# Two fused kernels in one stream: tile loops kept in the program instead of unrolled, and the state update formed in its own buffer

## What is computed

```python
m_new = np.maximum(f_gate[:, :, t] + m, i_gate[:, :, t])
f_stab = np.exp(f_gate[:, :, t] + m - m_new)
i_stab = np.exp(i_gate[:, :, t] - m_new)
C = f_stab[:, :, None, None] * C + i_stab[:, :, None, None] * np.einsum('bhd,bhe->bhde', vt, kt)
n = f_stab[:, :, None] * n + i_stab[:, :, None] * kt
h_tilde = np.einsum('bhde,bhe->bhd', C, qt)
y[:, :, t] = o * h_tilde / denom        # denom = max(|n.q|, 1), o = sigmoid(o_gate)
```

```python
xn = x / rms * rms_g
x = (silu(xn @ w_gate) * (xn @ w_val)) @ w_out      # first MLP
h = x @ w_in
out = (np.maximum(h, 0) + alpha * np.minimum(h, 0)) @ w_out2   # second MLP
```

## Time and profile before

| | us |
|---|---|
| median of 3 executions | 503.93 |
| all three | 505.44, 503.92, 503.93 |
| the profiled execution, its own device time | 505.44 |
| its span | 503.6 |

### The profile page before, as it was taken

One profiled execution on the slowest core, in us unless ns is written; L12 is line 12 of the kernel. 1 busy time (PEld: TensorE's weight loads), 2 busy tenths in 40 slices (PEclk: granted clock), 3 DMA queues, 4 the chain that ended last, 5 costly groups with the idle time before them and its releaser, 6 DMA issues.

```text
span 503.6 us, 9124 instructions
## 1 busy us (share of the span) xinstructions
PE 482.7 (96%) x3161; PEld 463.4 (92%) x3161; DVE 317.4 (63%) x643; ACT 212.7 (42%) x508; POOL 233.9 (46%) x250
## 2 busy tenths in 40 slices
PE   5998989999999999999999999999999999998996
PEld 3887978998999999998999999999899999988996
DVE  7585897657787474449678556438779622236663
ACT  1441536245635324236545423234654422245552
POOL 3540748535657326143746334340855522225673
PEclk9998999999999999999999999999999999999999
DMA  6768332123434680003344390002342320004562
GB/s 112 163 135 176 105 103 75 44 59 98 119 85 116 113 119 2 2 0 74 121 96 91 115 167 1 1 2 56 93 117 81 90 66 0 1 5 114 135 126 97
DMA packets 80729, 41.23 MB, mean 82 GB/s; under 512 B 51548, under 2 KB 80684, under 8 KB 80684
## 3 DMA queue, kind: packets, MB, share of 16 engines
q1 hardware_dynamic: 80684, 40.65, 36.2%
HBM read 38.67 MB, written 1.97 MB: 81 GB/s over the span
## 4 chain that ended last, share of the span: by engine, by line
PE 78%; DVE 12%; issue 3%; POOL 3%; ACT 3%; ACTq 0%; POOLq 0%; DVEq 0%
PE bank L976 38%; PE bank L984 16%; PE bank L987 8%; PE bank L940 4%; PE bank L928 3%; PE bank L904 2%; PE bank L881 2%; PE bank L935 2%; POOL w L837 1%; DVE u L750 1%; PE bank L946 1%; DVE xn L711 1%; PE bank L918 1%; PE bank L919 1%; DVE win L720 1%
## 5 line engine op out<-in xcount | busy, mean ns | idle before, releaser
L845 POOL TENSOR_TENSOR hidT<-hid,hidT 128x384 fp32r<-128x384 f32 x112 | 118.3, 1057 | 227.7 <-ACT hidT L510 227.4
L510 ACT CAST hidT<-hid 128x384 fp32r<-128x384 f32 x112 | 57.5, 513 | 131.5 <-DVE hid L733 93.8
L976 PE MATMUL bank<-x2T,win 128*128 128x384 f32 x512 | 100.2, 339 | 1.2 <-ACT x2T L551 0.8
L976 PEld LDWEIGHTS bank<-x2T,win 128*128 128x128 f32 x512 | 87.6, 188 | 2.9 <-DVE win L720 1.3
L727 DVE SCALAR_TENSOR_TENSOR u<-th,bank 128x384 f32<-128x384 f32 x48 | 26.6, 554 | 92.0 <-ACT th L532 91.9
L976 PE MATMUL bank<-xT,wg 128*128 128x384 f32 x384 | 76.4, 342 | 1.8 <-DVE u L727 1.8
L976 PE MATMUL bank<-xT,wv 128*128 128x384 f32 x384 | 76.3, 341 | 0.0
L984 PE MATMUL bank<-w,hidT 128*128 128x320 f32 x384 | 68.2, 313 | 4.1 <-POOL w L837 3.5
L976 PEld LDWEIGHTS bank<-xT,wg 128*128 128x128 f32 x384 | 67.1, 191 | 2.9 <-issue 2.0
L976 PEld LDWEIGHTS bank<-xT,wv 128*128 128x128 f32 x384 | 66.7, 189 | 1.2 <-DVE hid L733 0.4
L984 PEld LDWEIGHTS bank<-w,hidT 128*128 128x128 f32 x384 | 59.2, 188 | 6.9 <-POOL w L837 5.7
(11 more groups left out here) (126 smaller groups left out, 631.4 us busy)
## 6 DMA issues: line engine op xcount, KB each, us to landing
shared<-in_moe_w_out SPq DMA_DIRECT2D x38, 320.0 KB, 4.9
shared<-in_moe_w_in SPq DMA_DIRECT2D x34, 256.0 KB
shared<-in_moe_w_in SPq DMA_DIRECT2D x34, 128.0 KB
q_in<-in_q SPq DMA_DIRECT2D x12, 160.0 KB, 4.4
k_in<-in_k SPq DMA_DIRECT2D x12, 160.0 KB, 4.8
v_in<-in_v SPq DMA_DIRECT2D x12, 160.0 KB, 4.8
o_in<-in_o_gate SPq DMA_DIRECT2D x12, 160.0 KB, 4.4
shared<-in_moe_w_gate SPq DMA_DIRECT2D x6, 256.0 KB
```

What stands on the lines that cost most here:

```text
L510: a.copy(hidT[:, i % NH, 0], hid[:, i % 2]).then_inc(s_hid_hi, 1)
L845: gp.tensor_tensor(hidT[:, i % NH, 1], hid[:, i % 2], hidT[:, i % NH, 0].bitcast(F32), ALU.subtract).then_inc(s_hid_lo, 1)
L976: last = te.matmul(dst, w[:, blk, col:col + P], x[:, part, xb, :], start=(n == 0), stop=(n == len(terms) - 1))
```

## The change

Two things are changed.

- The loop over t = 1, 2 of every engine, and SP's loops over m in `stream`, become loops of the program (`Fori`): the body is there once, a register holds t or m, and a branch at its end goes back to its start. Every semaphore value and DMA address in it that depends on t or m is computed in registers.
- A new step on DVE, at the place of `state`: `upd` is the bank A[2] times `pairmask`, a constant of ones on each pair's own half and zeros on the cross blocks. The bank is free after it (`s_upd`), and PE's `kT` and one `xT` wait for that instead of `s_C`. In `inter` one add of `upd` into C takes the place of the two adds that read the bank. Four memsets fill `pairmask`.

```diff
--- before.py
+++ after.py
@@ -171,6 +171,8 @@
         C = sb("C", [P, H, DA])
         tmp = sb("tmp", [P, H, DA])
         hsum = sb("hsum", [P, H, DA])
+        upd = sb("upd", [P, H, DA])
+        pairmask = sb("pairmask", [P, 2, DA])
         den = sb("den", [P, 3, H])
         xr = sb("xr", [P, H, D])
         xa = sb("xa", [P, H, D])
@@ -268,6 +270,7 @@
         s_intra_mm = sem("s_intra_mm")
         s_hsum = sem("s_hsum")
         s_state_mm = sem("s_state_mm")
+        s_upd = sem("s_upd")
         s_C_dec = sem("s_C_dec")
         s_C = sem("s_C")
         s_absn = sem("s_absn")
@@ -310,7 +313,7 @@
         s_load_win = [sem(f"s_load_win{p}") for p in range(2)]
         s_load_w2 = [sem(f"s_load_w2{p}") for p in range(2)]
         s_group = [sem(f"s_group{g}") for g in range(G)]
-        N_CONST, N_CONST_DVE, GATE_STEPS = 14, 12, 3 * G + 6
+        N_CONST, N_CONST_DVE, GATE_STEPS = 14, 16, 3 * G + 6
 
 
 
@@ -330,7 +333,7 @@
 
             walk(PROLOGUE, mlp, att, weights, None, 0)
             walk(FIRST, mlp, att, weights, 0, 1)
-            for t in range(1, NT - 1):
+            with eng.Fori(1, NT - 1) as t:
                 walk(MERGED, mlp, att, weights, t, t + 1)
             walk(EPILOGUE, mlp, att, weights, NT - 1, None)
 
@@ -409,7 +412,7 @@
 
             def stream(t):
 
-                for m in range(J2 // 4 - 1):
+                with sp.Fori(0, J2 // 4 - 1) as m:
                     for p in range(2):
                         load_w2(t, 2 * m + p, p)
                         load_win_behind(t, 2 * m + p, p, 2 * m + p + 2)
@@ -447,7 +450,7 @@
                 load_win(p, p)
             stream(0)
             store(0)
-            for t in range(1, NT - 1):
+            with sp.Fori(1, NT - 1) as t:
                 load_rows(t + 1)
                 for g in range(G):
                     load_group(t + 1, g)
@@ -601,6 +604,9 @@
             vec.memset(cap[:, ::HALVES], -BIG).then_inc(s_const_dve, 1)
             for r in (64, 96):
                 vec.memset(decay_lhs[r:r + H, :].bitcast(F32), 1.0).then_inc(s_const_dve, 1)
+            for r, one in ((0, 0), (REM, 1)):
+                vec.memset(pairmask[r:r + REM, one], 1.0).then_inc(s_const_dve, 1)
+                vec.memset(pairmask[r:r + REM, 1 - one], 0.0).then_inc(s_const_dve, 1)
             vec.memset(win[0:REM, :, NB, :].bitcast(F32), 0.0).then_inc(s_const_dve, 1)
             dve.wait_ge(s_const, N_CONST)
             vec.tensor_copy(identR[:, :], ident[:, :]).then_inc(s_const_dve, 1)
@@ -676,12 +682,9 @@
                     dve.wait_ge(s_gx, BACK + t + 1)
                     vec.tensor_tensor(tmp[:, :, :], heads(A[1]), wide(gx[:, 0, g], P, H, DA), ALU.mult).then_inc(s_tmp, 1)
                     vec.tensor_tensor(C[0:KP], C[0:KP], wide(gx[0:KP, 2, g], KP, H, DA), ALU.mult).then_inc(s_C_dec, 1)
-                    dve.wait_ge(s_state_mm, BACK + n + 1)
+                    dve.wait_ge(s_upd, n + 1)
                     dve.wait_ge(s_C_dec, n + 1)
-                    for half in range(2):
-                        own = slice(HP * half, HP * half + D)
-                        last = vec.tensor_tensor(C[own, half::2], C[own, half::2], heads(A[2])[own, half::2], ALU.add)
-                    last.then_inc(s_C, 1)
+                    vec.tensor_tensor(C[0:KP], C[0:KP], upd[0:KP], ALU.add).then_inc(s_C, 1)
                 elif what == "intra":
                     dve.wait_ge(s_intra_mm, BACK + n + 1)
                     dve.wait_ge(s_tmp, n + 1)
@@ -696,6 +699,11 @@
                     vec.tensor_scalar(den[:, 1, :], den[:, 0, :], 1.0, None, ALU.max).then_inc(s_den, 1)
                     dve.wait_ge(s_den, n + 1)
                     vec.reciprocal(den[:, 2, :], den[:, 1, :]).then_inc(s_rden, 1)
+                elif what == "state":
+                    dve.wait_ge(s_state_mm, BACK + n + 1)
+                    dve.wait_ge(s_C, BACK + n)
+                    vec.tensor_tensor(upd[0:KP, :, :].rearrange("p (a b) d -> p a (b d)", b=2), heads(A[2])[0:KP].rearrange("p (a b) d -> p a (b d)", b=2),
+                                      mid(pairmask[0:KP, :, :].rearrange("p b d -> p (b d)"), KP, PAIRS, 2 * DA), ALU.mult).then_inc(s_upd, 1)
                 elif what == "norm":
                     dve.wait_ge(s_rden, n + 1)
                     dve.wait_ge(s_xr, BACK + n + 1)
@@ -898,7 +906,7 @@
                     if what == "qT":
                         pe.wait_ge(s_x_lo, BACK + n - 2) if g == 0 else pe.wait_ge(s_tmp, n)
                     else:
-                        pe.wait_ge(s_gate_step, GATE_STEPS * (t + 1)) if g == 0 else pe.wait_ge(s_C, BACK + n)
+                        pe.wait_ge(s_gate_step, GATE_STEPS * (t + 1)) if g == 0 else pe.wait_ge(s_upd, n)
                     src, bank_ = (q_in, A[1]) if what == "qT" else (k_in, A[2])
                     for c in range(PAIRS):
                         last = te.transpose(bank_[0:KP, c * CH:(c + 1) * CH],
@@ -954,7 +962,7 @@
                     elif g == 0:
                         pe.wait_ge(s_tmp, G * t + G)
                     elif g == 1:
-                        pe.wait_ge(s_C, BACK + G * t + G)
+                        pe.wait_ge(s_upd, G * t + G)
                     else:
                         pe.wait_ge(s_hsum, G * t + G)
                     for c in range(XB):
```

## The result

| | before | after |
|---|---|---|
| median of the runs, us | 504.13 (4 runs, 503.92 to 505.44) | 508.68 (4 runs, 507.23 to 510.04) |
| the profiled execution | 505.44, span 503.6 | 508.86, span 507.1 |

The account below looks back on a forecast made before the run. PE was taken to bound the tiles and DVE to pace the opening; memsets 0.4 + group 1 0.3 + branch 2.7 + registers 0.3 = 3.7 us over the 503.93 median gave 507.6, range 504.4 to 510.6.

Parts of the forecast that it names:

- The bound: Whole kernel: PE bounds the tiles, so its stops add in full and DVE's additions there cost nothing; DVE paces the opening.
- The memsets: DVE's constants in the opening: four mask memsets, uncovered, delay PE's first matmul and the gate rows by 0.4 us (0.2 to 0.5).
- Group 1: Opening's second group: `upd` shifts the decay, and the new add may meet POOL's work; +0.3 us, from 0 to +0.8.
- The two DVE terms: Opening: the mask's memsets at +0.4 us and the state update in group 1 at +0.3 us.
- The bank's earlier release: PE's next `kT` waits for `s_upd`, some 1.5 us earlier than `s_C`; gain 0.
- The branch: Between tiles 1 and 2: PE's instruction fetch takes 3.5 us less 0.8 of work in hand, a 2.7 us stop (0 to 4.2).
- rival (a): At PE's branch: the loop's start is still held; 504.4 us lies inside it, and it shares the 0.21 for the same speed.
- The registers: PE's tile loop: 91 sequencer instructions a round, mostly covered by the queue running ahead; +0.3 us, from 0 to 6.6.
- Rival (c): PE's tile loop: register instructions are not covered behind waits; half exposed costs +3.3 us, 510.6, all 513.9; chance 0.10.
- rival (b): Tile 2: the granted clock falls after PE's stop at the branch, 1.7 us more, 509.3; chance 0.17.
- Rival (d): Opening's 1.75 us half-clock loss falls away and the branch is free: 503.2, or 502.4 with lower DVE terms; chance 0.04.
- What is late next: At the branch: the other engines' fetches are covered by PE's stop, and come late if PE does not stop.

Follow-up runs that it names:

- e_upd_only: B with the change's new state update and mask but no loops; 504.27 us, ratio 0.9991.
- e_pe_slot0: B with only PE's tile loop kept, its first instruction at slot 0 of a 256-instruction packet; 504.44 us, ratio 1.0001.
- B: The kernel before the change; its 23 executions beside each batch lie near 503.9 us (lower level) or near 505.5 us (upper level).
- e_stop: B, unrolled, with PE's first matmul of tile 2 waiting for six more DVE memsets; 509.03 us, ratio 1.0084.
- e_change_slot0: The whole change with PE's tile loop at slot 0 and 20 instead of 12 keep matmuls ending the opening; 508.02 us, ratio 1.0056.
- e_loop_only: B with all the loops of the change and the old state update; 509.71 us, ratio 1.0093.
- e_pe_loop: B with only PE's tile loop kept in the program, all other engines unrolled; 508.33 us, ratio 1.0078.
- e_others_loop: B with the tile loops of DVE, ACT and POOL only, PE and SP unrolled; 503.78 us, ratio 0.9994.
- e_pe_slot200: B with only PE's tile loop kept, its first instruction at slot 200 of a 256-instruction packet; 508.24 us, ratio 1.0076.
- e_pe_hint: B with only PE's tile loop kept and a prefetch hint for its branch; 504.63 us, ratio 1.0001.
- e_keep20: B with 20 instead of 12 keep matmuls ahead of the opening's last transposes; 503.89 us, ratio 0.9986.

## Why the prediction came out as it did

**The bound** was read rightly. PE is busy in the tiles to within 1 us, so a stop of PE is added in full, and DVE's additions there vanish: `e_upd_only` puts 12 longer groups on DVE and costs 0.3 us.

**The memsets**: +0.4 us forecast, 0.24 measured at the gate rows (5.49 to 5.25). The lower bound named the reason: they overlap. The first two start 0.05 us apart, though each takes 0.09 us, as worked out.

**Group 1**: +0.3 forecast. `upd` takes 492 ns, `tmp` and the decay are moved, the decay loses less to POOL (0.92 instead of 1.33 us), and the new add is stretched instead (0.83): as described, except that POOL was not done where the forecast took it to be. Its `kw` follows `wv` at once (at 29.37 in the trace of before, at 29.82 here), and it is `kw` that meets the add. `hsum` is 0.73 late, 0.24 of it from the start, so the group costs 0.49. But 0.39 of the 0.73 are regained by the end of the opening (44.75 against 44.41), where the chain waits for others as well. The two DVE terms, 0.7 together, are 0.3 in the whole kernel. They were sized at the place and not at the end of the stage.

**The bank's earlier release**: no gain is seen, as forecast; it was not measured apart from the rest of the update.

**The branch**: 2.7 forecast, 2.79 measured, 2.88 and 3.02 in the two kernels with PE's loop unplaced. The forecast took a DMA of 8 KB as the nearest row for a fetch, less the 0.8 us in hand, and that was near. It is in part luck: no row shows when PE's queue reached the branch, so neither of the two parts is confirmed. What it could not read from the rows is that the cost hangs on the placement: rival (a) is true of `e_pe_slot0`, word for word ("if more than six packets are held, a body of 1555 + 91 instructions still is"), and false of the change. That its loop starts elsewhere in a packet was not read off; it follows from placing the loop being enough to take the stop away and to bring it back. The argument asked how many packets are held and not where in a packet the body begins.

**The registers**: 0.3 forecast, at most 0.1. Rival (c) is out.

**The step that failed** is the choice between the forecast and rival (b). The terms as measured, on B's lower level, make 503.9 + 0.3 + 2.8 = 507.0; three of the ten executions lie there, from 507.08 to 507.23. With the clock's fall it is 507.0 + 1.6 = 508.6: the median of the four runs is 508.68, the profiled one 508.86, and three of ten lie there. The other four, 509.28 to 510.04, are 0.7 to 1.4 us above that sum. No profile of one of them is kept; a longer stretch at half clock, as in `e_stop`, where it costs 1.1 us more than one of 3.4, would have about that size. The term of 1.7 was sized rightly from the earlier trace rows (1.57 measured) and given a chance of 0.17, where seven of ten executions have this loss or more. The reason given against it, that PE had worked in pieces ahead of the earlier gap and works without a break here, was a guess with no row behind it; the row at hand, a stop of 1.99 us with half clock behind it, spoke for it. The predicted 507.6 is only 1.1 us under the median because the DVE terms and the registers were 0.6 too high in sum while 1.6 was left out: that the number came near is in part errors that cancel.

**Rival (d)** has a slip in its sum: with the DVE terms at their lower ends, 0.2 and 0, its 503.2 becomes 502.7 and not 502.4. Its first condition is true and was not seen as a term of its own: the update shortens the opening's last wait, and the 1.6 us between the two levels of B is saved in the executions that had it (`e_upd_only`: none of twelve at the upper level). The medians hardly show it, since B's lies at the lower level in most comparisons.

**What is late next**: the prediction said that the other engines' fetches come late if PE does not stop. `e_change_slot0` shows just that, at 2.34 us and half a clock, and I had left it out when I expected that kernel to return to 504.4.

## What to carry to other kernels

A loop kept in the program costs nothing in itself on an engine that is the bound; its backward branch costs a stop of 2.4 to 3.0 us here when the body's start is no longer held, so count the body and its offset in packets, place it or use the hint, and do it on every engine whose next result is wanted at once, not on the slowest alone (of the engines, only PE's loop was placed here; the hint was tried on all four). Price a stop of TensorE of the lengths seen here, 2.3 to 3.3 us, as the stop plus the half-clock stretch behind it, and look in the profile of before for a short stop of which this is already true. A few useless matmuls in the last gap of a stage bought 1.6 us in those executions, 9 to 11 of 23, that lie at the upper level.

## What the runs showed of the hardware

- A body of 1646 instructions on PE is held across its backward branch from slot 0 of a packet and lost from slot 200 (0 and 9 packets in tile 2; 504.44 and 508.24 us). The stop is 2.44 to 3.02 us in four kernels.
- Stops of 2.34 to 3.34 us are followed by 3.4 to 3.5 us (once 6.8) at a granted clock of 0.50 to 0.54 in five profiles, whether a branch, a semaphore or a late DVE result caused them; one such stretch costs 1.6 us where PE is the bound. One stop, of 3.02 us, was followed by full clock. The opening's gap of 1.98 to 2.00 us has the fall behind it in two profiles (B and `e_loop_only`) and full clock in six (`e_pe_loop`, `e_others_loop`, `e_stop`, `e_pe_slot0`, `e_pe_slot200`, `e_pe_hint`). What decides between the two was not found.
- A half-clock stretch where PE waits for DVE costs nothing: the window of `e_keep20` below has PE at 0.50, at a time of 503.89 us, and B has full clock there.

```profile
63.70:67.10 3.40, 3.40 (x13) 3.40 (x12) 3.29 (x8) 1.83 (x4) 1.28 (x1) 0.50 0.29 73
```

- DVE's operation over two SBUF tensors is stretched while POOL works (the new add in the change: 0.50 us in the eight groups in which POOL does nothing beside it, 0.83 to 0.97 in the four in which POOL works); the one that reads a bank is not (500 ns at most in 12, eight of them beside POOL).
